# Attention on one core: pooled and local scores in turn on PE, even keys ahead of the normalising on GpSimd, tails in fours

## The chip, the cores and the metric

The kernel runs on one core of a Trainium2 chip. The metric is the device time of one execution in microseconds (us); lower is better.

## What is computed

Attention over 4 x 8 heads of 576 positions and 64 channels, then two dense layers over the 2304 tokens, all in float32. This change is in the attention.

```python
q_d = q.reshape(B, H, Sd, factor, D).mean(axis=3)      # factor = 4, Sd = 144; k_d, v_d too
out_d = sm_attn(q_d, k_d, v_d)                         # pooled: softmax over all 144 keys
out_up = np.repeat(out_d, factor, axis=2)
mask = np.abs(pos[:, None] - pos[None, :]) < factor    # local: keys at most 3 away
scores = np.where(mask, scale * np.matmul(q, k.transpose(0, 1, 3, 2)), -1000000000.0)
...
return (out_up + out_local).astype(np.float32)
```

The first layer is `(h * tanh(softplus(h))) @ w_out` with `h = x @ w_in` (512 to 2048 and back), the second a softmax-gated unit with layer norm (512 to 1024 and back).

## The kernel before, in words

Each engine has its program written out by hand, in the order in which it runs; semaphores tie them together. The attention works on 16 units, each a pair of heads of one batch: head 0 lies in partitions 0 to 63, head 1 in 64 to 127. All engines loop over u = 0 to 15 (PE and ACT two more), and the attention ends where PE takes up `hidden(0, ...)`, the first layer (L919).

- **SP** starts all loads, in one queue. In step s it sends for v of unit s - 2 (the values, 512 first positions, `v4`), in even s also the tails of two units (the last 64 positions, 16 partitions, `vt4`), then queries and keys of unit s (`qkT`, three buffers), then the windows of unit s - 3 (`vw`, the values of the local part). Each load first waits until its buffer is free: v until the values of two units earlier are pooled (`pool_v`), the tails until the pair before is (`pool_vt`).
- **POOL** (GpSimd) does in iteration u: `normalise_local(u - 1)` (L683, waits for `rden_ok`), queries of unit u + 1 and, if that is even, its keys (`pool_queries_keys`, L656 and L658: add pairs into `half_qk`, then add the halves), the values of unit u (`pool_values`, L666 and L668) and in even u the tails of u and u + 1 (`pool_two_tails`, L674 and L676). Steps of one pooling are chained by `own`, which waits for the engine's own last operation.
- **PE** in iteration u: `turn_local(u - 2)` (L851, needs that unit normalised), `turn_pooled(u - 2)` (L861, L866), `score_pooled(u)` (L819, six products of 64x144, one for each of three query blocks and two heads), `score_local(u)` (L832 masks, L838 twenty products of 64x64), then `value_pooled(u - 2)` (L878 with vd, L883 with the tails vdt) and `value_local(u - 2)` (L899). In units 0 and 1 the local scores come first. The local blocks are in two groups, jp = 0 and jp = 1 (the first and the second blocks); `half_rows(h, jp)` puts head h of the first blocks in the output rows of h, of the second blocks in those of the other head. The pooled scores go to the output rows of h.
- **DVE** in iteration u: pooled maxima (L1494, waits for `p_scored`), local maxima and subtraction (L1503, L1510, waits for `l_scored`), in even u the keys of the odd unit u + 1 (L1468), in odd u the eviction of a local output (L1532), sums (L1517) and the reciprocals `rden` (L1526). In iterations 3, 7 and 11 it also adds the pooled output (L1548), in 4, 8 and 12 it splits off a low part (L1554).
- **ACT**: copies of the turned parts (L1161, L1166), `normalise_pooled` (L1150), `exp_pooled` (L1141), `exp_local` (L1171), evictions.

After attention the layers run on PE without a gap; they are not touched.

## Time and profile before

| | us |
|---|---|
| median of 3 runs | 689.97 |
| lowest, highest | 688.26, 690.58 |
| the profiled execution | 683.98 |
| its span | 682.2 |
| PE busy in the span | 664.3 (97%) |
| DVE, ACT, POOL busy | 422.3, 325.7, 282.2 |

The profile is of one execution, whose own time is 683.98 us; busy time is per engine, and in 97% of the span PE works. The clock granted to PE was full (1.00) throughout. Start times below are counted from the start of the span.

### The profile page before, as it was taken

What the parts mean: (1) busy time and instruction counts of PE and PEld (TensorE: products, weight loads), DVE (VectorE), ACT (ScalarE), POOL (GpSimd) and SP (SyncE); (2) the same over time, 40 slices, a digit from 0 to 9 for tenths busy, and PEclk for the clock granted to TensorE, in tenths of its full rate; (3) what the DMA queues carried; (4) which work ended last, traced back from release to release, by engine and by line L of the source; (5) the groups of instructions that cost most, each with busy time, mean ns of one, the idle gap of its engine ahead of it and who ended that gap; (6) DMA issues with size and microseconds to landing.
All of it is one profiled execution on the core that took longest, in us unless ns stands there. A gap on an engine that the chain in (4) does not pass through costs nothing.

```text
span 682.2 us, 13003 instructions
## 1 busy us (share of the span) xinstructions
PE 664.3 (97%) x5002; PEld 570.3 (84%) x5002; DVE 422.3 (62%) x763; ACT 325.7 (48%) x687; POOL 282.2 (41%) x342
## 2 busy tenths in 40 slices
PE   5999999999999999999999999999999999999998
PEld 4777778888998989999899988888778888888886
DVE  7999859545765566555544322455787556855671
ACT  5999962343454366443442211137365454445432
POOL 6999803020795437554000000586355333542100
PEclk9999999999999999999999999999999999999999
DMA  8989791000000000000200001012100000000001
GB/s 263 255 269 271 184 369 38 0 1 1 1 0 1 1 1 1 1 1 1 62 2 1 1 0 61 1 32 63 31 16 16 31 32 31 1 32 31 32 17 47
DMA packets 26115, 37.54 MB, mean 55 GB/s; under 512 B 2512, under 2 KB 12742, under 8 KB 26054
## 3 DMA queue, kind: packets, MB, share of 16 engines
q1 hardware_dynamic: 26054, 36.71, 17.3%
q8 instruction: 40, 0.66, 0.4%
q14 instruction: 21, 0.17, 0.1%
HBM read 31.98 MB, written 4.72 MB: 54 GB/s over the span
## 4 chain that ended last, share of the span: by engine, by line
PE 91%; DVE 2%; ACT 2%; issue 2%; POOL 2%; DMA 0%; SPq 0%; ACTq 0%; POOLq 0%; DVEq 0%
PE psum L967 29%; PE psum L919 16%; PE psum L1080 14%; PE psum L1057 12%; PE psum L953 12%; PE psum L1066 2%; PE psum L819 1%; PE psum L851 1%; POOL prob L683 1%; PE psum L899 1%; PE psum L838 1%; PE psum L861 1%; PE psum L866 0%; ACT pprob L1141 0%; PE psum L878 0%
## 5 line engine op out<-in xcount | busy, mean ns | idle before, releaser
L967 PE MATMUL psum<-ghi,whi 128*128 128x512 f32 (+1 forms) x320 | 118.2, 370 | 0.0
L967 PE MATMUL psum<-glo,whi 128*128 128x512 f32 (+1 forms) x320 | 118.1, 369 | 0.0
L967 PE MATMUL psum<-ghi,wlo 128*128 128x512 f32 (+1 forms) x320 | 117.7, 368 | 0.0
L1216 ACT ACTIVATE g_sb<-psum 128x512 f32<-128x512 f32 (+1 forms) x48 | 25.3, 527 | 135.5 <-PE psum L919 134.7
L1598 DVE CAST ghi<-g_sb 128x512 fp32r<-128x512 f32 (+1 forms) x48 | 23.5, 490 | 102.2 <-PE psum L967 87.2
L919 PE MATMUL psum<-xhi,whi 128*128 128x512 f32 (+1 forms) x256 | 85.6, 365 | 0.5 <-ACT g_sb L1216 0.3
L1603 DVE TENSOR_TENSOR glo<-g_sb,ghi 128x512 fp32r<-128x512 f32 (+1 forms) x80 | 66.2, 828 | 19.6 <-ACT ghi L1242 18.0
L967 PEld LDWEIGHTS psum<-ghi,wlo 128*128 128x128 f32 x320 | 60.3, 189 | 10.3
L967 PEld LDWEIGHTS psum<-ghi,whi 128*128 128x128 f32 x320 | 60.5, 189 | 9.7 <-issue 0.4
L919 PE MATMUL psum<-xlo,whi 128*128 128x512 f32 (+1 forms) x192 | 68.0, 354 | 0.0
L967 PEld LDWEIGHTS psum<-glo,whi 128*128 128x128 f32 x320 | 60.5, 189 | 8.8
L953 PE MATMUL psum<-ahi,flo 128*128 128x256 f32 x224 | 63.4, 283 | 0.0
L953 PE MATMUL psum<-ahi,fhi 128*128 128x256 f32 x224 | 63.2, 282 | 0.0
L1080 PE MATMUL psum<-whi,lhi 128*128 128x512 f32 x144 | 56.4, 392 | 0.9 <-DVE llo L1757 0.9
L1080 PE MATMUL psum<-whi,llo 128*128 128x512 f32 x144 | 56.1, 389 | 0.0
L1080 PE MATMUL psum<-wlo,lhi 128*128 128x512 f32 x144 | 56.0, 389 | 0.0
L919 PEld LDWEIGHTS psum<-xhi,whi 128*128 128x128 f32 x256 | 48.3, 189 | 8.3 <-ACT g_sb L1216 0.4
L709 POOL TENSOR_TENSOR fsum<-wraw 128x256 f32<-128x256 f32 x16 | 12.3, 769 | 97.5 <-PE psum L953 35.9
L1057 PE MATMUL psum<-whi,yhi 128*128 128x512 f32 x126 | 50.8, 403 | 0.1
L1211 ACT ACTIVATE g_sb<-g_sb 128x512 f32<-128x512 f32 x32 | 20.2, 630 | 61.1 <-DVE g_sb L1654 61.1
L1057 PE MATMUL psum<-wlo,yhi 128*128 128x512 f32 x126 | 49.3, 391 | 0.0
L1057 PE MATMUL psum<-whi,ylo 128*128 128x512 f32 x126 | 49.1, 389 | 0.0
(175 smaller groups left out, 1607.2 us busy)
## 6 DMA issues: line engine op xcount, KB each, us to landing
wraw<-w_dram SPq DMA_DIRECT2D x12, 512.0 KB, 7.9
qkT<-qT_dram SPq DMA_DIRECT2D x16, 288.0 KB, 3.6
qkT<-kT_dram SPq DMA_DIRECT2D x16, 288.0 KB, 5.0
out_dram<-ob SPq DMA_DIRECT2D x18, 256.0 KB, 2.0
vw<-v_dram SPq DMA_DIRECT2D x15, 280.0 KB
v<-v_dram SPq DMA_DIRECT2D x16, 256.0 KB, 4.7
wraw<-w_dram SPq DMA_DIRECT2D x16, 256.0 KB, 7.1
b<-w_dram SPq DMA_DIRECT2D x4, 512.0 KB, 4.2
```

The lines of the kernel that those rows point to most:

```text
L683: nc.gpsimd.tensor_tensor(rows, rows, rden[:, par, 0:NB].unsqueeze(2).broadcast_to([P, NB, KW]), ALU.mult).then_inc(l_norm, 1)
L709: nc.gpsimd.tensor_tensor(to[:, 0], raw_block(j, 0, 1), raw_block(j, 0, 0), ALU.subtract).then_inc(ft_ok, 1)
L919: ins = nc.tensor.matmul(bank, a[:, kdx, :], b[:, kdx, 0:size], start=(kdx == 0 and n == 0), stop=(kdx == KD - 1 and n == 2))
L953: ins = nc.tensor.matmul(bank, a, b, start=(k == 0 and m == 0), stop=(k == KH - 1 and m == 2))
L967: ins = nc.tensor.matmul(psum[:, YB + m, 0:size], a[:, w], b[:, (t * F1 + f) % GR, 0:size], start=(f == 0 and n == 0), stop=(f == F1 - 1 a ...
L1057: ins = nc.tensor.matmul(bank, a[p % 2][:, n, k, :], b, start=(k == 0 and m == 0), stop=(k == KH - 1 and m == 2))
L1066: ins = nc.tensor.transpose(psum[:, T2B + c // 4, (c % 4) * P:(c % 4 + 1) * P], so[:, par, c * P:(c + 1) * P], ident[:])
L1080: ins = nc.tensor.matmul(bank, a[:, par, c, :], b[:, w], start=(c == 0 and n == 0), stop=(c == F2 - 1 and n == 2))
L1211: nc.scalar.activation(g_sb[:, f % HR, :], g_sb[:, f % HR, :], ACT.Mish).then_inc(g_ok, 1)
L1216: nc.scalar.activation(g_sb[:, f % HR, 0:size], psum[:, HB1 + f % HB, 0:size], ACT.Mish).then_inc(g_ok, 1)
L1598: nc.vector.tensor_copy(ghi[:, (t * F1 + f) % GR, 0:size], g_sb[:, f % HR, 0:size]).then_inc(ghi_ok, 1)
L1603: nc.vector.tensor_tensor(glo[:, (t * F1 + f) % GR, 0:size], g_sb[:, f % HR, 0:size], ghi[:, (t * F1 + f) % GR, 0:size].bitcast(F32), ALU. ...
```

## The change

On PE, units 2 to 15 get their scores from one function, `score_both`: masks of the second blocks, then pooled and local products of the second blocks in turn, then masks and products of the first blocks. It waits for all its inputs at its start. On GpSimd, keys are pooled apart from queries, and in odd iterations ahead of the normalising (in iteration 1 behind it); tails are pooled for four units at once (32 partitions each, 16 of them filled), so their products on PE use 32 rows instead of 64. The values of unit 1 are pooled in iteration 2, the first tails in iteration 1. SP sends for queries and keys ahead of the values; four tails are sent for at the start, and later two of them in each of the steps 3, 4, 7, 8, 11 and 12, the first two behind a wait for the tails before.

The diff. In `score_both` the inner functions `masked(jp)`, `local(i, jp, h)` and `pooled(b, h)` are left out; each issues the same product, with the same operands, as its line in `score_local` or `score_pooled`.

```diff
--- before.py
+++ after.py
@@ -42,6 +42,8 @@
 PR = HD + PB
 PS = 2 * HD
 PT = POOLED - P
+FOUR = 4
+QP = P // FOUR
 QPAD = (NPB - 1) * PB + HD
 
 SEQP = SEQ + 12
@@ -559,26 +561,33 @@
 
 
 
+            def load_tails(u, n):
+                for i in range(u, u + n):
+                    at = i % FOUR * QP
+                    tail = v_d[i][POOLF * P:SEQ].rearrange("(p t) c -> p (t c)", t=POOLF)
+                    sp.dma_start(vt4[at:at + PT, :], tail).then_inc(ld_vt4, 16)
+
             for s in range(UNITS + 3):
+                if s < UNITS:
+                    wait(sp, l_scored, s + 1 - RQ)
+                    wait(sp, p_scored, s + 1 - RQ)
+                    sp.dma_start(qkT[:, s % RQ, 0, 0:SEQ], qT_d[s]).then_inc(ld_qk[s % RQ], 16)
+                    sp.dma_start(qkT[:, s % RQ, 1, 0:SEQ], kT_d[s]).then_inc(ld_qk[s % RQ], 16)
                 if 1 < s < UNITS + 2:
                     u = s - 2
                     wait(sp, pool_v, u - 1)
                     sp.dma_start(v4[:, u % 2, :], v_d[u][0:POOLF * P].rearrange("(p t) c -> p (t c)", t=POOLF))\
                       .then_inc(ld_v4[u % 2], 16)
-                    if u == 0:
-                        sp.wait_ge(rest_ok, 2)
-                    if u % 2 == 0:
-                        wait(sp, pool_vt, u // 2)
-                        for h in range(2):
-                            tail = v_d[u + h][POOLF * P:SEQ].rearrange("(p t) c -> p (t c)", t=POOLF)
-                            sp.dma_start(vt4[h * HD:h * HD + PT, :], tail).then_inc(ld_vt4, 16)
-                if s < UNITS:
-                    wait(sp, l_scored, s + 1 - RQ)
-                    wait(sp, p_scored, s + 1 - RQ)
-                    sp.dma_start(qkT[:, s % RQ, 0, 0:SEQ], qT_d[s]).then_inc(ld_qk[s % RQ], 16)
-                    sp.dma_start(qkT[:, s % RQ, 1, 0:SEQ], kT_d[s]).then_inc(ld_qk[s % RQ], 16)
+                if s == 2:
+                    sp.wait_ge(rest_ok, 2)
+                    load_tails(0, FOUR)
                 if s > 2:
                     load_windows(s - 3)
+                if s > 2 and s % FOUR == FOUR - 1 and s + 1 < UNITS:
+                    sp.wait_ge(pool_vt, (s + 1) // FOUR)
+                    load_tails(s + 1, 2)
+                if s > 2 and s % FOUR == 0 and s < UNITS:
+                    load_tails(s + 2, 2)
                 if s in W_IN:
                     load_w_in(0, W_IN.index(s))
             for kdx in range(KD):
@@ -644,19 +653,24 @@
                                     base=0, pattern=[[KW, 2], [1, KW]], channel_multiplier=-1).then_inc(band_ok, 1)
             own(nc.gpsimd.memset(mhalf[:], -0.5))
 
-            def pool_queries_keys(u):
-                par = u % 2
+            def pool_two_adds(u, a, dst, ok):
+                halves = half_qk[:, a].rearrange("p (i r) -> p i r", r=2)
+                four = qkT[:, u % RQ, a, 0:SEQ].rearrange("p (i r) -> p i r", r=4)
+                own(nc.gpsimd.tensor_tensor(halves, four[:, :, 0:2], four[:, :, 2:4], ALU.add))
+                nc.gpsimd.tensor_tensor(dst[:, u % 2, 0:POOLED], halves[:, :, 0], halves[:, :, 1], ALU.add)\
+                  .then_inc(ok, 1)
+
+            def pool_queries(u):
                 pool.wait_ge(ld_qk[u % RQ], 32 * (u // RQ + 1))
                 wait(pool, p_scored, u - 1)
                 wait(pool, pool_q, u)
-                wait(pool, pool_k[0], (u + 1) // 2)
-                n = 1 if u % 2 else 2
-                halves = half_qk[:].rearrange("p a (i r) -> p a i r", r=2)
-                four = qkT[:, u % RQ, :, 0:SEQ].rearrange("p a (i r) -> p a i r", r=4)
-                own(nc.gpsimd.tensor_tensor(halves[:, 0:n], four[:, 0:n, :, 0:2], four[:, 0:n, :, 2:4], ALU.add))
-                for a, dst in enumerate((qd, kd)[:n]):
-                    nc.gpsimd.tensor_tensor(dst[:, par, 0:POOLED], halves[:, a, :, 0], halves[:, a, :, 1],
-                                            ALU.add).then_inc((pool_q, pool_k[0])[a], 1)
+                pool_two_adds(u, 0, qd, pool_q)
+
+            def pool_even_keys(u):
+                pool.wait_ge(ld_qk[u % RQ], 32 * (u // RQ + 1))
+                wait(pool, p_scored, u - 1)
+                pool.wait_ge(pool_k[0], u // 2)
+                pool_two_adds(u, 1, kd, pool_k[0])
 
             def pool_values(u):
                 par = u % 2
@@ -667,13 +681,13 @@
                 wait(pool, p_valued, u - 1)
                 nc.gpsimd.tensor_tensor(vd[:, par, :], half_v[:, 0:P], half_v[:, P:2 * P], ALU.add).then_inc(pool_v, 1)
 
-            def pool_two_tails(u):
-                two = u // 2
-                pool.wait_ge(ld_vt4, 32 * (two + 1))
-                wait(pool, pool_vt, two)
+            def pool_four_tails(u):
+                four = u // FOUR
+                pool.wait_ge(ld_vt4, 16 * FOUR * (four + 1))
+                wait(pool, pool_vt, four)
                 own(nc.gpsimd.tensor_tensor(half_vt[:], vt4[:, 0:2 * P], vt4[:, 2 * P:4 * P], ALU.add))
-                wait(pool, p_valued, u - 2)
-                nc.gpsimd.tensor_tensor(vdt[:, two % 2, :], half_vt[:, 0:P], half_vt[:, P:2 * P], ALU.add)\
+                wait(pool, p_valued, u - FOUR)
+                nc.gpsimd.tensor_tensor(vdt[:, four % 2, :], half_vt[:, 0:P], half_vt[:, P:2 * P], ALU.add)\
                   .then_inc(pool_vt, 1)
 
             def normalise_local(u):
@@ -684,14 +698,22 @@
                                         ALU.mult).then_inc(l_norm, 1)
 
             for u in range(UNITS + 1):
+                if u % 2 == 1 and 2 < u + 1 < UNITS:
+                    pool_even_keys(u + 1)
                 if u > 0:
                     normalise_local(u - 1)
-                if 0 < u + 1 < UNITS:
-                    pool_queries_keys(u + 1)
-                if u < UNITS:
+                if u == 1:
+                    pool_even_keys(2)
+                if u + 1 < UNITS:
+                    pool_queries(u + 1)
+                if u == 1:
+                    pool_four_tails(0)
+                elif u < UNITS:
+                    if u == 2:
+                        pool_values(1)
                     pool_values(u)
-                    if u % 2 == 0:
-                        pool_two_tails(u)
+                    if u > 0 and u % FOUR == 0:
+                        pool_four_tails(u)
                 if u == UNITS - 1:
                     pool.wait_ge(wi_hi, 2)
                     nc.gpsimd.tensor_tensor(first_low(1), in_piece(wraw, 1), first_high(1).bitcast(F32),
@@ -840,6 +862,49 @@
                                                    start=False, stop=(i == NP - 1))
                 ins.then_inc(l_scored, 1)
 
+            def score_both(u):
+
+                par = u % 2
+                qk = qkT[:, u % RQ].rearrange("p a s -> p (a s)")
+                pe.wait_ge(ld_qk[u % RQ], 32 * (u // RQ + 1))
+                pe.wait_ge(l_sub, u)
+                pe.wait_ge(pool_q, u + 1)
+                pe.wait_ge(pool_k[par], u // 2 + 1)
+                pe.wait_ge(p_exp, u)
+
...
+                masked(1)
+                for i in range(NP):
+                    for h in range(2):
+                        if i < NPB:
+                            ins = pooled(i, h)
+                            if (i, h) == (NPB - 1, 1):
+                                ins.then_inc(p_scored, 1)
+                        local(i, 1, h)
+                masked(0)
+                for i in range(NP):
+                    for h in range(2):
+                        ins = local(i, 0, h)
+                ins.then_inc(l_scored, 1)
+
@@ -860,7 +925,7 @@
                     at = b * PS
                     nc.tensor.transpose(turned[:, at:at + PR], pprob[0:PR, par, b, 0:P], ident[0:PR, 0:PR])
 
-                k0 = P - par * HD
+                k0 = P - u % FOUR * QP
                 for b in range(NPB):
                     at = TP1 + b * PS
                     ins = nc.tensor.transpose(turned[0:POOLED - k0, at:at + PR], pprob[0:PR, par, b, k0:POOLED],
@@ -871,8 +936,8 @@
                 par = u % 2
                 pe.wait_ge(p_copied, u + 1)
                 pe.wait_ge(pool_v, u + 1)
-                pe.wait_ge(pool_vt, u // 2 + 1)
-                half = slice(par * HD, (par + 1) * HD)
+                pe.wait_ge(pool_vt, u // FOUR + 1)
+                part = slice(u % FOUR * QP, (u % FOUR + 1) * QP)
                 for h in range(2):
                     rows = slice(h * HD, (h + 1) * HD)
                     nc.tensor.matmul(turned[rows, OD0:OD0 + POOLED], vd[:, par, rows], pprobT[:, 0, :, h, :],
@@ -880,8 +945,8 @@
 
                 for h in range(2):
                     rows = slice(h * HD, (h + 1) * HD)
-                    ins = nc.tensor.matmul(turned[rows, OD0:OD0 + POOLED], vdt[half, u // 2 % 2, rows],
-                                           pprobT[half, 1, :, h, :], start=False, stop=True)
+                    ins = nc.tensor.matmul(turned[rows, OD0:OD0 + POOLED], vdt[part, u // FOUR % 2, rows],
+                                           pprobT[part, 1, :, h, :], start=False, stop=True)
                 ins.then_inc(p_valued, 1)
 
             def value_local(u):
@@ -978,12 +1043,11 @@
                 if u >= LATE:
                     turn_local(u - LATE)
                     turn_pooled(u - LATE)
-                if u < UNITS:
-                    if u >= FIRST:
-                        score_pooled(u)
+                if u < FIRST:
                     score_local(u)
-                    if u < FIRST:
-                        score_pooled(u)
+                    score_pooled(u)
+                elif u < UNITS:
+                    score_both(u)
 
                 if u == UNITS:
                     pe.wait_ge(l_sub, UNITS)
```

The order of instructions. First POOL, from the values of unit 1 (before) and the tails of units 0 to 3 (now) to the normalising of unit 2. In the names half_v and vd are values, half_vt and vdt tails, qd and kd pooled queries and keys, `prob<-prob,rden` is a normalising. Before:

```order
L666 TENSOR_TENSOR half_v<-v_58 128x256 [waits pool_v,ld_v4_1]
L668 TENSOR_TENSOR vd<-half_v 128x128 [waits pool_own]
L683 TENSOR_TENSOR prob<-prob,rden 128x640 [waits rden_ok]
L656 TENSOR_TENSOR half_qk<-qkT 128x288 [waits pool_q,pool_k0,p_scored,ld_qk0]
L658 TENSOR_TENSOR qd<-half_qk 128x144 [waits pool_own]
L666 TENSOR_TENSOR half_v<-v_58 128x256 [waits pool_v,ld_v4_0]
L668 TENSOR_TENSOR vd<-half_v 128x128 [waits p_valued,pool_own]
L674 TENSOR_TENSOR half_vt<-vt_59 128x256 [waits pool_vt,ld_vt4]
L676 TENSOR_TENSOR vdt<-half_vt 128x128 [waits pool_own]
L683 TENSOR_TENSOR prob<-prob,rden 128x640 [waits rden_ok]
```

and now:

```order
L688 TENSOR_TENSOR half_vt<-vt_59 128x256 [waits ld_vt4]
L690 TENSOR_TENSOR vdt<-half_vt 128x128 [waits pool_own]
L697 TENSOR_TENSOR prob<-prob,rden 128x640 [waits rden_ok]
L659 TENSOR_TENSOR half_qk<-qkT 128x288 [waits pool_q,p_scored,ld_qk0]
L660 TENSOR_TENSOR qd<-half_qk 128x144 [waits pool_own]
L680 TENSOR_TENSOR half_v<-v_58 128x256 [waits pool_v,ld_v4_1]
L682 TENSOR_TENSOR vd<-half_v 128x128 [waits pool_own]
L680 TENSOR_TENSOR half_v<-v_58 128x256 [waits pool_v,ld_v4_0]
L682 TENSOR_TENSOR vd<-half_v 128x128 [waits p_valued,pool_own]
L659 TENSOR_TENSOR half_qk<-qkT 128x288 [waits pool_k0,p_scored,ld_qk1]
L660 TENSOR_TENSOR kd<-half_qk 128x144 [waits pool_own]
L697 TENSOR_TENSOR prob<-prob,rden 128x640 [waits rden_ok]
```

The values of unit 1 come behind the first normalising of these (unit 1) and directly ahead of those of unit 2; there are no tails between; and the keys of unit 4 stand ahead of the normalising of unit 2 instead of behind it.

Second, SP's queue from the last window load of unit 0 on (v_58 values, vt_59 tails). Before:

```order
L537 DMA vw<-v_dram 6x5x128
L566 DMA v_58<-v_dram 128x512 [waits pool_v]
L574 DMA vt_59<-v_dram 16x512 [waits pool_vt]
L574 DMA vt_59<-v_dram 16x512
L578 DMA qkT<-qT_dram 128x576 [waits p_scored,l_scored]
L579 DMA qkT<-kT_dram 128x576
L537 DMA vw<-v_dram 112x5x128
```

and now:

```order
L539 DMA vw<-v_dram 6x5x128
L568 DMA vt_59<-v_dram 16x512 [waits pool_vt]
L568 DMA vt_59<-v_dram 16x512
L574 DMA qkT<-qT_dram 128x576 [waits p_scored,l_scored]
L575 DMA qkT<-kT_dram 128x576
L579 DMA v_58<-v_dram 128x512 [waits pool_v]
L539 DMA vw<-v_dram 112x5x128
```

The values of unit 2 were next behind the windows; now they are behind two tails, which wait for `pool_vt`, and behind queries and keys of unit 4.

## Rows read from the trace of the kernel before

**Rows 1.** Windows, 20 us of attention and 20 us of the first layer.

```profile
core 0: us, PE busy (x) PEld busy (x) DVE busy (x) ACT busy (x) POOL busy (x), PEclk, DMA share, GB/s
40.00:60.00 20.00, 18.45 (x504) 15.57 (x495) 18.78 (x40) 18.80 (x60) 19.21 (x28) 1.00 0.87 249
120.00:140.00 20.00, 20.00 (x90) 16.57 (x89) 9.40 (x18) 6.36 (x12) 0.00 (x0) 1.00 0.01 1
```

**Rows 2.** Timeline of POOL: start us, us, engine, line, operation, out<-in, count.

```profile
47.40 0.82 POOL L668 TENSOR_TENSOR vd<-half_v 128x128 f32<-128x128 f32 x1
48.19 0.73 POOL L674 TENSOR_TENSOR half_vt<-vt 128x256 f32<-128x256 f32 x1
...
49.41 1.26 POOL L683 TENSOR_TENSOR prob<-prob,rden 128x640 f32<-128x640 f32 x1
50.62 1.15 POOL L656 TENSOR_TENSOR half_qk<-qkT 128x576 f32<-128x576 f32 x1
...
52.23 0.42 POOL L658 TENSOR_TENSOR kd<-half_qk 128x144 f32<-128x144 f32 x1
...
53.83 1.26 POOL L683 TENSOR_TENSOR prob<-prob,rden 128x640 f32<-128x640 f32 x1
55.05 0.67 POOL L656 TENSOR_TENSOR half_qk<-qkT 128x288 f32<-128x288 f32 x1
...
56.17 0.73 POOL L666 TENSOR_TENSOR half_v<-v 128x256 f32<-128x256 f32 x1
```

**Rows 3.** Timeline of DVE over units 9 to 11.

```profile
53.31 0.24 DVE L1526 RECIPROCAL rden<-dsum 128x13 f32<-128x13 f32 x1
53.75 0.61 DVE L1494 TENSOR_REDUCE psum<-psum 128x3 f32<-128x432 f32 x1 [0.19 <-PE psum L819]
...
58.12 0.24 DVE L1526 RECIPROCAL rden<-dsum 128x13 f32<-128x13 f32 x1
58.28 0.55 DVE L1494 TENSOR_REDUCE psum<-psum 128x3 f32<-128x432 f32 x1
...
63.02 0.24 DVE L1526 RECIPROCAL rden<-dsum 128x13 f32<-128x13 f32 x1
```

**Rows 4.** Timeline of PE, its iteration 11.

```profile
55.72 0.77 PE L851 MATMUL psum<-ident,prob 128*128 128x128 f32 x5
...
57.00 0.71 PE L819 MATMUL psum<-kd,qd 64*64 64x144 f32 x8
...
57.53 0.42 PE L819 MATMUL psum<-kd,qd 64*64 64x144 f32 x4
...
58.60 0.47 PE L878 MATMUL psum<-pprobT,vd 128*64 128x144 f32 x4
59.00 0.34 PE L883 MATMUL psum<-pprobT,vdt 64*64 64x144 f32 x2
59.01 0.38 PE L899 MATMUL psum<-probT,vw 64*64 64x58 f32 x5
...
59.96 0.77 PE L851 MATMUL psum<-ident,prob 128*128 128x128 f32 x5
```

**Rows 5.** Timeline of SP's queue, the load of unit 2's values.

```profile
10.69 0.36 SPq L566 DMA_DIRECT2D v<-v_dram  x1
```

**Rows 6.** Timeline of POOL, first and third normalising.

```profile
10.87 1.26 POOL L683 TENSOR_TENSOR prob<-prob,rden 128x640 f32<-128x640 f32 x1
...
20.09 1.26 POOL L683 TENSOR_TENSOR prob<-prob,rden 128x640 f32<-128x640 f32 x1
```

**Rows 7.** Timeline of DVE, pooled maxima of unit 4.

```profile
24.88 0.62 DVE L1494 TENSOR_REDUCE psum<-psum 128x3 f32<-128x432 f32 x1 [0.16 <-PE psum L819]
```

**Rows 8.** The loads of tile v, from issue to landing.

```profile
DMA to landing us min/median/max: 3.4/4.7/7.3
```

**Rows 9.** Timeline of POOL, normalising of unit 12.

```profile
68.66 1.26 POOL L683 TENSOR_TENSOR prob<-prob,rden 128x640 f32<-128x640 f32 x1
```

**Rows 10.** Timeline of PE, end of attention, where unit 14 is turned.

```profile
80.52 0.33 PE L899 MATMUL psum<-probT,vw 64*64 64x58 f32 x7 [1.00 <-issue]
80.78 0.77 PE L851 MATMUL psum<-ident,prob 128*128 128x128 f32 x5
```

16 lines of the change are left out of this document (added).

## The prediction

> **What bounds the kernel now.** I read the windows first, then the timelines of GpSimd (POOL), VectorE (DVE) and PE through a few units, then the start and the end of attention. The windows say where a change of attention can count: in the first layer PE is busy 20.00 of 20 us, in attention no engine is, but POOL has 19.21, ACT 18.80, DVE 18.78 and PE 18.45 [rows 1]. After attention PE never waits for long, so the program ends earlier or later by the amount by which PE gets earlier or later to the turning of unit 14, at 80.78 us [rows 10].
>
> Inside attention POOL is the pace-maker. Its operations follow one another with no idle time; normalising starts at 49.41 for unit 8 and 68.66 for unit 12, so four units take 19.25 us [rows 2, 9]. DVE is close behind: the reciprocals of unit 10 end at 58.12 + 0.24 = 58.36, 4.61 after that unit's pooled maxima started (53.75), those of unit 11 at 63.26, 4.90 later, and each time POOL comes for them within 0.3 us [rows 3]. Now the maxima of an even unit wait for PE, and PE for POOL: the even keys are ready 3.24 us after normalising began (49.41 to 52.65), and the maxima start 4.34 after it [rows 2, 3].
>
> **GpSimd's work.** From start to start: normalising N 1.22 (53.83 to 55.05); halving and pooling one of queries or keys 1.12 (55.05 to 56.17); tails T 1.22 (48.19 to 49.41), and values V the same, as the shapes are [rows 2]. Before, the even unit's half over both took 1.15 and its two second steps 0.4 each, 2.03 together (50.62 to 52.65); apart they are 2 x 1.12 = 2.24, so the split costs 0.2 per even unit. Tails by fours save 1.22 per four units. Per four units that is 0.4 more and 1.2 less: POOL needs 0.8 less, 18.4. DVE can't follow so far: 18.78 of 20 busy is 18.1 of 19.25, and its two short waits for ACT's exponentials stay, so 18.1 to 18.7 is its floor (estimate). Were work alone the limit, 0.5 to 1.1 per four units would be won.
>
> **The new loop.** The even keys now stand ahead of the normalising, and PE turns a unit (which needs it normalised) ahead of the next scores. So the order adds 1.12 to the wait of the turning. From a normalising's start to the maxima two units on: 1.26, 0.05 to PE, 1.28 turning (55.72 to 57.00), 0.95 pooled scores (57.00 to 57.95), 0.04 = 3.58 [rows 2, 4]. Every fourth unit has the tails just ahead of the even keys. From the reciprocal before them: 0.07, N + query + V + T 4.78, a block of 0.37 (vd at 47.40 took 0.82 where a slightly wider kd took 0.42 [rows 2]; this recurs in such a unit, with DVE's work beside it), even keys 1.12, 3.58 to the maxima, 4.61 and 4.90 to the two next reciprocals: 19.43. That is 0.18 more than the 19.25 of now. So I expect the saved work to become a wait of POOL for reciprocals ahead of the tails, with a late normalising behind them: little won or lost in the steady part, +0.4 over the two such loops from unit 4 to 12.
>
> **The start.** SP is one queue. In its step 3 it now waits for the first tails to be pooled, before unit 4's queries and keys and unit 2's values are sent for. The first normalising is at 10.87 [rows 6]; behind it stand even keys, queries and tails, 1.22 + 1.12 + 1.12 + 1.22, so the wait ends at 15.55. Then come two tails and two other loads, 0.36 [rows 5] to 0.5 us each, and unit 2's values go out at about 17.25 (10.69 before [rows 5]). Values land 3.4 to 4.7 after issue, 7.3 at worst [rows 8]: at 20.7 to 22.0, I take 21.3 because the queue has run empty. POOL wants them at 15.55 + N + query + V = 19.1, and unit 4's keys and the normalising of unit 2 stand behind them: it starts at 21.3 + 1.22 + 1.12 = 23.65 instead of 20.09 [rows 6]. Unit 4's maxima follow at +3.58 = 27.2 instead of 24.88 [rows 7]: 2.3 late. Windows for unit 1 are sent for later too, and come at about the same time as this, so they hide. POOL then reaches unit 4's normalising at 23.65 + 3.56 + 0.4 (a block) + 4.78 + 0.37 + 1.12 = 33.9, and two loops bring unit 12's to 72.8, 4.1 after the 68.66 of now [rows 9].
>
> **PE.** The pooled scores use the diagonal pairs of row and column halves, and of the local ones the second blocks use the other two. Both groups already overlap, and the diagonal ones carry pooled, mask and first blocks whatever the order: 57.00 to 58.60, 1.60 [rows 4]. In turn they may shorten this by up to 0.15, or delay the last pooled product by up to 0.2, if the loads between them cost time; I take nothing for both. The new waits ahead of the pooled scores (scores subtracted, local queries and keys) are fulfilled before PE comes to them in either order.
>
> The tail product is the other edit on PE. Its tile goes from 64 rows to 32. Now the switch from vd (128 rows) to vdt (64) takes 58.60 to 59.00, 0.40, and then the local values start beside vdt at 59.01, in the same 64 x 64 shape [rows 4]. With 32 rows both sides of vdt differ, so I charge a second 0.35 per unit (bounds 0, and the 0.40 of the row). The Trainium skill (TensorEngine Tiling (Array Packing), Key Properties) says that changing the tiling mode, not just the tile, drains TensorE; the trace agrees, with the 0.40 between 58.60 and 59.00 and none before 59.01. Inside the loop PE has that to spare: two units take 9.2 of 9.6. At the end it has not.
>
> **The end.** There are no tails at unit 14 any more, and POOL is no longer last. PE is: 1.31 after unit 12's normalising starts it turns unit 12, and two iterations of 4.24 (55.72 to 59.96 [rows 4]) + 0.35 later it turns unit 14, at 72.8 + 10.5 = 83.3. Now it is 80.78, and that holds a pause of 1.00 inside the local values which no semaphore explains [rows 10]. +2.5 if it doesn't recur, +3.5 if it does. I take +2.9.
>
> **The sum.** Start +2.3 at unit 4's maxima; +1.4 more by unit 12's normalising, which is the late place behind the tails, and +0.4 of the loops; end -1.2 with what PE adds: +2.9. The profiled execution is 683.98 us for a span of 682.2, and becomes 686.9; the median of the runs shown, 689.97, lies 6.0 above it, and becomes 692.9.
>
> **Rivals.** (1) *The start stays late and the steady part runs at DVE's pace.* If normalising never gets late behind the tails (shorter turning, POOL blocked less) a loop is 18.7, two win 1.1, and the missing tails of unit 14 another 1.0: +2.3 - 2.1 = +0.2, 690.2. For it: POOL's work is 18.4. Against: the sum of 19.43 has only measured terms. Chance 0.30. (2) *Faster.* The mechanism is the same relief of POOL, without the late values. It decides at POOL's second values in its iteration 2: if unit 2's values are there by 19.1, nothing is lost, and -2.1 to -2.4 remains, 687.7. Against it: issue at 17.25 would need a landing in 1.9 us, and the quickest was 3.4 [rows 8]; only an earlier end of the first tails would do. Chance 0.12. (3) *Starved loads.* In steps 7 and 11 SP again waits for the tails, and the values of units 6, 10 and 14 are sent behind that wait, about 3 us later than now, with some 5 us left against landings of 4.7 and up to 7.3 [rows 8]. One more microsecond each: +3 on the forecast, 695.9. Chance 0.13. The forecast has 0.45. That the interleaving does nothing for the time is part of all four.
>
> **How the numbers follow.** About 0.3%, 2.07 us, is what can be told from no change: below 687.9 faster, above 692.0 slower. The forecast's own range is 691.3 to 694.5 (values landing at 3.4 or 4.7, pause or none, second switch 0 or 0.40), some four fifths of it above 692.0. With rival 3, that gives slower 0.52; faster 0.12; the rest, rival 1 and the lower part of the forecast, 0.36. The range of 8 in 10 leaves out rival 2 and the far part of rival 3: 688.2 to 695.6.
>
> **What would show it.** Right: POOL idle before unit 2's values by some 2 us, released by a load; normalising of unit 2 near 23.6, of unit 12 near 72.8; short idles of POOL on reciprocals before the iterations with tails; maxima of even units 3.6 after normalising instead of 4.3; vdt and the local values no longer starting together; pooled scores ended 0.95 after their start. Wrong: no load in POOL's idle time at the start, four units in 18.7, or unit 14 turned by 81.

## The result and the profile after

| | before | after |
|---|---|---|
| median, runs on the same chip | 687.1 (9 runs) | 692.98 (9 runs) |
| lowest, highest | 684.39, 690.58 | 690.16, 695.74 |
| the profiled execution | 683.98 | 690.16 |
| its span | 682.2 | 688.3 |
| pooled maxima of unit 4 | 24.88 | 28.64 |
| normalising of units 4, 8, 12 | 30.13, 49.41, 68.66 | 35.21, 54.89, 75.17 |
| turning of unit 14 | 80.78 | 86.54 |

Ratio 1.0101, 95% interval 1.0078 to 1.0123: slower by 6.9 us (5.4 to 8.5). The two medians of the table are only 5.9 apart. Three of the nine runs of before are those shown ahead of the prediction (689.97, 688.26, 690.58), among the slowest; the other six have a median of 686.2, and from there it is 6.8.

The forecast's sign and its 692.9 us came true, but the second only by chance. It was +2.9 on the profiled execution, where +6.2 was measured; and before itself, in this comparison, has a median of 687.1 and not the 689.97 from which the forecast started. A loss of 0.4% was foreseen, and 1.0% came.

The windows of the changed kernel first, with the columns of [rows 1].

```profile
core 0: us, PE busy (x) PEld busy (x) DVE busy (x) ACT busy (x) POOL busy (x), PEclk, DMA share, GB/s
40.00:60.00 20.00, 18.65 (x468) 14.92 (x466) 18.32 (x39) 18.23 (x58) 17.74 (x27) 1.00 0.92 248
120.00:140.00 20.00, 20.00 (x90) 16.57 (x89) 11.79 (x22) 6.50 (x12) 0.00 (x0) 1.00 0.00 0
```

POOL has become lighter, 17.74 of 20 us instead of 19.21, and nothing was won by it. The first layer is as full as it was, so the difference again stands in the turning of unit 14, +5.76 of the +6.1 in the span. Here is the end of attention on PE (timeline, as in [rows 10]), with three more places where PE stopped or was stopped. The last number in brackets is the idle time before a row, and behind the arrow stands what ended it; "issue" means that the profile shows nothing that ended it.

```profile
12.58 0.77 PE L916 MATMUL psum<-ident,prob 128*128 128x128 f32 x5 [1.61 <-POOL prob L697]
...
14.99 0.47 PE L879 MATMUL psum<-maskb,identb 64*64 64x320 bf16 x2 [1.07 <-POOL qd L660]
...
17.97 0.45 PE L943 MATMUL psum<-pprobT,vd 128*64 128x144 f32 x2
...
54.11 0.68 PE L884 MATMUL psum<-qkT 64*64 64x64 f32 x17 [1.06 <-issue]
...
81.74 0.46 PE L964 MATMUL psum<-probT,vw 64*64 64x58 f32 x17 [1.01 <-issue]
...
86.54 0.66 PE L916 MATMUL psum<-ident,prob 128*128 128x128 f32 x4
```

Next come three views of the start: SP's queue from step 3 on (compare [rows 5], where unit 2's values go out at 10.69), POOL's timeline ([rows 6, 9]), and the maxima of unit 4 on DVE ([rows 7]).

```profile
16.02 0.79 SPq L568 DMA_DIRECT2D vt<-v_dram  x2
16.91 0.37 SPq L574 DMA_DIRECT2D qkT<-qT_dram  x1
17.32 0.43 SPq L575 DMA_DIRECT2D qkT<-kT_dram  x1
17.80 0.43 SPq L579 DMA_DIRECT2D v<-v_dram  x1
```

```profile
10.05 0.72 POOL L680 TENSOR_TENSOR half_v<-v 128x256 f32<-128x256 f32 x1 [1.56 <-DMA v<-v_dram]
...
15.54 0.46 POOL L690 TENSOR_TENSOR vdt<-half_vt 128x128 f32<-128x128 f32 x1
...
22.23 0.73 POOL L680 TENSOR_TENSOR half_v<-v 128x256 f32<-128x256 f32 x1 [2.67 <-DMA v<-v_dram]
...
24.57 1.26 POOL L697 TENSOR_TENSOR prob<-prob,rden 128x640 f32<-128x640 f32 x1
25.79 1.11 POOL L659 TENSOR_TENSOR half_qk<-qkT 128x288 f32<-128x288 f32 x1
...
68.56 1.26 POOL L697 TENSOR_TENSOR prob<-prob,rden 128x640 f32<-128x640 f32 x1 [0.98 <-DVE rden L1590]
...
71.28 0.73 POOL L680 TENSOR_TENSOR half_v<-v 128x256 f32<-128x256 f32 x1 [0.33 <-DMA v<-v_dram]
...
75.17 1.26 POOL L697 TENSOR_TENSOR prob<-prob,rden 128x640 f32<-128x640 f32 x1
```

```profile
28.64 0.62 DVE L1558 TENSOR_REDUCE psum<-psum 128x3 f32<-128x432 f32 x1 [1.04 <-PE psum L890]
```

What to see: the first tails are pooled at 15.54 + 0.46 = 16.00, SP takes up its queue at 16.02, and unit 2's values leave at 17.80. POOL then stands for 2.67 until they are there. Later waits for values are small: four after 23 us, of 0.23 to 0.56 (0.33 at 71.28 is one).

The same stretch in windows, changed kernel, then the kernel before, shows a thing that the forecast hadn't in it.

```profile
14.00:16.00 2.00, 1.01 (x25) 1.04 (x29) 0.42 (x2) 2.00 (x6) 1.84 (x5) 0.71 0.02 6
16.00:18.00 2.00, 2.00 (x40) 1.81 (x34) 0.78 (x2) 0.50 (x4) 1.92 (x3) 0.50 0.17 42
18.00:20.00 2.00, 2.00 (x54) 1.53 (x53) 1.88 (x4) 1.23 (x7) 1.48 (x3) 0.94 0.94 288
```

```profile
14.00:16.00 2.00, 1.77 (x59) 1.74 (x60) 1.17 (x5) 1.98 (x5) 1.92 (x4) 1.00 0.93 297
16.00:18.00 2.00, 2.00 (x56) 1.74 (x55) 1.97 (x5) 1.63 (x8) 1.92 (x4) 1.00 1.10 277
```

While SP waits the DMA engines are empty (0.02 instead of 0.93). In the same stretch the clock granted to PE falls to 0.50, which is 1.2 GHz, after PE had waited 1.61 for the first normalising and 1.07 for unit 2's queries. Unit 2's scores take 14.99 to 17.97, 2.98 us, instead of 1.60 [rows 4].

What brings the clock down there isn't shown, and it isn't SP's wait alone. Between 12 and 18 us seven of the fourteen traces of this document have a window of 2 us at 0.50 to 0.56: the changed kernel, e2, e3, e4, e7, e9 and e11. Three of them, e2, e7 and e9, have no wait of SP in step 3, and e9 is the kernel before with nothing but the scores in turn. PE's two waits don't decide it either: they are 0.94 and 1.07 both in e3, where the clock fell to 0.53, and in e5, where it stayed at 1.00; in the kernel before they are 1.34 and 0.70, at 1.00.

### The profile page after: what moved, and what is told of

It reads as the page before. It is cut to its first block, busy times and chain, and to the rows that moved or that the text cites. A ratio compares the mean times of both kernels' runs of the same rounds, so it can differ in the third digit from the quotient of the medians.

```text
span 688.3 us, 12986 instructions
## 1 busy us (share of the span) xinstructions
PE 667.7 (97%) x5002; PEld 571.2 (83%) x5002; DVE 424.4 (62%) x763; ACT 326.1 (47%) x687; POOL 278.3 (40%) x341
## 4 chain that ended last, share of the span: by engine, by line
PE 86%; POOL 8%; DVE 2%; issue 2%; DMA 1%; ACT 1%; SPq 0%; POOLq 0%; ACTq 0%; DVEq 0%
PE psum L1032 29%; PE psum L984 16%; PE psum L1144 13%; PE psum L1121 12%; PE psum L1018 12%; POOL prob L697 2%; PE psum L1130 2%; POOL half_qk L659 2%; POOL half_v L680 1%; DMA v<-v_dram 1%; POOL vd L682 1%; POOL qd L660 1%; PE psum L916 1%; PE psum L964 0%; POOL half_vt L688 0%
```

## The experiments

All ratios are to the kernel before, run beside them.

| run | what it is | ratio | 95% interval |
|---|---|---|---|
| after | the changed kernel | 1.0101 | 1.0078 to 1.0123 |
| e1_late_tails | without SP's wait ahead of the values | 1.0038 | 1.0020 to 1.0057 |
| e2_two_tails | tails by twos | 1.0043 | 1.0025 to 1.0061 |
| e3_keys_behind | even keys behind the normalising | 1.0076 | 1.0053 to 1.0098 |
| e4_scores_apart | scores not in turn | 1.0104 | 1.0076 to 1.0133 |
| e5_start_mended | e1, and values ahead of queries on SP | 1.0029 | 1.0007 to 1.0052 |
| e6_mended_filler | e5, and filler products on PE | 1.0013 | 0.9997 to 1.0030 |
| e7_combined | e5, and even keys behind the normalising | 1.0031 | 1.0012 to 1.0050 |
| e8_only_keys | before, with keys split and even keys ahead | 1.0015 | 0.9994 to 1.0036 |
| e9_only_scores | before, with scores in turn | 1.0004 | 0.9984 to 1.0025 |
| e10_only_fours | before, with tails by fours and keys split | 1.0025 | 1.0005 to 1.0045 |
| e11_changed_filler | the changed kernel, with filler products | 1.0078 | 1.0055 to 1.0101 |
| e12_before_filler | before, with filler products | 0.9997 | 0.9973 to 1.0020 |

### SP's wait (e1)

```diff
-                if s > 2 and s % FOUR == FOUR - 1 and s + 1 < UNITS:
-                    sp.wait_ge(pool_vt, (s + 1) // FOUR)
-                    load_tails(s + 1, 2)
                 if s > 2 and s % FOUR == 0 and s < UNITS:
-                    load_tails(s + 2, 2)
+                    sp.wait_ge(pool_vt, s // FOUR)
+                    load_tails(s, FOUR)
```

> The changed kernel, but SP sends for the next four tails in one piece at the end of steps 4, 8 and 12, behind the values and windows of that step, instead of two of them behind a wait at the end of steps 3, 7 and 11. Theory A (the wait in SP's step 3 makes unit 2's values late, and the delay lasts): GpSimd no longer idles 2.7 us for them, the pooled maxima of unit 4 start near 25.1 instead of 28.6 us, and 3 to 3.5 us of the 6 to 7 are given back: ratio to before 1.003 to 1.006. Theory B (the start is made up anyway; the loss is in the loops and in PE's pauses): the start moves, the end does not, ratio 1.008 or more.

Measured: 688.79 against 685.97, ratio 1.0038. SP's queue, and POOL's timeline, of this kernel:

```profile
13.04 0.43 SPq L579 DMA_DIRECT2D v<-v_dram  x1
...
15.75 1.72 SPq L568 DMA_DIRECT2D vt<-v_dram  x4
```

```profile
19.45 0.73 POOL L678 TENSOR_TENSOR half_v<-v 128x256 f32<-128x256 f32 x1
...
21.80 1.26 POOL L695 TENSOR_TENSOR prob<-prob,rden 128x640 f32<-128x640 f32 x1
```

Unit 2's values go out at 13.04 instead of 17.80, POOL pools them at 19.45 without a wait for a load, and unit 2 is normalised at 21.80 instead of 24.57. Between the two ratios lie 0.63%, 4.3 us: the wait of SP for the tails is the larger part of the loss. The mean granted clock of the runs, too, is nearer to that of before (0.9973; before 0.9982, changed kernel 0.9942). The two kernels were not run in the same comparison, so the 4.3 us have the width of both intervals, some 2 us on either side.

The profiled execution shows less of it. Unit 4's maxima are at 25.95 (near 25.1 was expected, 28.64 in the changed kernel), but unit 14 is turned at 84.55 instead of 86.54, 2.0 earlier. It holds a wait of 1.07 for values at 69.25, and the clock granted from 76 to 78 us was 0.50.

### Tails by twos (e2)

In the changed kernel the loads, the pooling and the products of the tails are those of before; SP's new order of queries and values, the early keys and the scores in turn stay.

Of its edit, the part in POOL's loop:

```diff
-                if u == 1:
-                    pool_four_tails(0)
-                elif u < UNITS:
-                    if u == 2:
-                        pool_values(1)
+                if u < UNITS:
                     pool_values(u)
-                    if u > 0 and u % FOUR == 0:
-                        pool_four_tails(u)
+                    if u % 2 == 0:
+                        pool_two_tails(u)
```

> The changed kernel with tails by twos again (loads, pooling, 64-row products), everything else as changed. GpSimd then has 18.9 us of own work per four units and 0.8 of blocks, 19.7, more than the 19.25 of before. Theory A: the start is as before (maxima of unit 4 at 25 to 25.5), the loops are 19.7, ratio 1.002 to 1.004. Theory B (keys ahead of the normalising, scores in turn or pauses cost the most): ratio 1.007 or more.

Measured: ratio 1.0043. This also takes away SP's wait, and by the ratio it gives back as much as e1 does. Its loops of four units take 19.8 us each, as foreseen (normalising at 34.83, 54.62 and 74.41). Its trace does not show the start that was expected: unit 4's maxima are at 28.41, not at 25 to 25.5. In this execution the granted clock was 0.64, 0.50, 0.50 and 0.65 in the windows from 14 to 22 us, and POOL waited 1.87 for the reciprocals of unit 3, until 28.57. How the start ran in its other executions isn't known. Once SP's wait is away, fours and twos can't be told apart (1.0038 against 1.0043): the pooling of tails saved on POOL bought nothing that can be measured.

### Even keys behind the normalising (e3)

```diff
-                if u % 2 == 1 and 2 < u + 1 < UNITS:
-                    pool_even_keys(u + 1)
                 if u > 0:
                     normalise_local(u - 1)
-                if u == 1:
-                    pool_even_keys(2)
+                if u % 2 == 1 and u + 1 < UNITS:
+                    pool_even_keys(u + 1)
```

> The changed kernel with the even keys behind the normalising again (still apart from the queries). Theory A: the start stays late by 3.5 us or more, and a loop gets 0.2 shorter (maxima 4.5 after normalising against 1.12 + 3.58): ratio 1.008 to 1.010. Theory B (the late normalising behind the tails is most of the loss): ratio 1.006 or less.

Measured: ratio 1.0076, 1.7 us less than the changed kernel, though the intervals overlap. In the trace unit 2 is normalised at 23.30 instead of 24.57, since the keys of unit 4 (1.12) no longer stand between the late values and it. That piece is a cost of the order only where POOL has been held up; e7 below puts the same edit on the mended start. The ratio fell between the two theories (1.008 to 1.010, and 1.006 or less). The start did stay late (maxima of unit 4 at 28.38), but the trace does not show loops shorter by 0.2: the two take 20.67 and 19.71, together 40.4, against 40.0 in the changed kernel.

### Scores apart (e4)

```diff
-                if u < FIRST:
-                    score_local(u)
-                    score_pooled(u)
-                elif u < UNITS:
-                    score_both(u)
+                if u < UNITS:
+                    if u >= FIRST:
+                        score_pooled(u)
+                    score_local(u)
+                    if u < FIRST:
+                        score_pooled(u)
```

> The changed kernel with pooled scores ahead of all local scores again. My theory: no difference in time, since scoring takes 1.60 to 1.62 us in both orders: ratio 1.009 to 1.011 as for the changed kernel. Rival: taking turns brings PE's pauses of 1.0 us (four or more of them against one before) or the low clock at unit 2; then they go, and the ratio is 1.007 or less.

Measured: ratio 1.0104, against 1.0101 with the scores in turn. No difference can be told. Its profiled execution was an unlucky one (granted clock 0.989 on average, a pause of 1.50 us on PE ending at 24.80), and its start times are therefore not compared. The low clock at unit 2 (0.50 from 16 to 18 us) came without the turns as well, and the ratio did not fall, so the rival falls.

### Start mended altogether (e5), filler products (e6), keys behind (e7)

e5 is e1 with SP's loads of queries and keys behind that of the values again:

```diff
-                if s < UNITS:
-                    ...
-                    sp.dma_start(qkT[:, s % RQ, 1, 0:SEQ], kT_d[s]).then_inc(ld_qk[s % RQ], 16)
                 if 1 < s < UNITS + 2:
                     ...
+                if s < UNITS:
+                    ...
+                    sp.dma_start(qkT[:, s % RQ, 1, 0:SEQ], kT_d[s]).then_inc(ld_qk[s % RQ], 16)
```

> The kernel of e1 (tails of four sent for behind windows), and SP sends for values ahead of queries and keys again, as before the change. What e1 left of the start is GpSimd's 1.6 us wait for unit 0's values and 0.5 to 1.1 us waits for later ones. Theory A: those waits go, and another 1 us is given back: ratio 1.002 to 1.003. Rival (the rest is the loops' order and the low clock): 1.0035 to 1.0045.

e6 adds four products that nobody reads, ahead of unit 2's scores:

```diff
                 elif u < UNITS:
+                    if u in (2,):
+                        for i in range(4):
+                            nc.tensor.matmul(psum[:, OB, 320:448], ident[:], ident[:], start=True, stop=True)
                     score_both(u)
```

> The kernel of e5 with four products of the identity with itself (0.2 us each at full clock) on PE, written to unused columns, ahead of unit 2's scores, so that PE works where it waits for unit 2's queries. Clock theory: the clock, which fell to its low level at about 15 us in four of five profiles of changed kernels and in none of before, stays at 1.00, unit 2's scores take 1.6 us instead of 3, and the time falls by 1 to 1.7 us against e5. Rival: the clock falls as often, or later, and the time is that of e5 within 0.5 us.

e7 is e5 with the edit of e3.

> The kernel of e5 with the even keys behind the normalising, as in e3. The start is as before, and GpSimd's work is 18.5 us per four units, with a loop of 19.1 behind the tails by my sum, no tails at unit 14. Theory A (the loop of late normalising is real, 0.3 us and more per four units): faster than e5 by 1 to 2 us, ratio 1.000 or below. Rival (position of the keys hardly matters; the shorter work of GpSimd does not reach the end): ratio that of e5.

Measured: 688.29, 687.03 and 688.86 against 686.26; ratios 1.0029, 1.0013 and 1.0031. In e5 the maxima of unit 4 are at 25.28, 0.4 behind those of before, and the first normalising at 10.54: the 1.56 us for which POOL stood ahead of unit 0's values are gone. Yet some 2 us stay. The keys ahead of the normalising or behind it make no difference now (1.0029, 1.0031). e6 had a granted clock of 1.00 in 7 of its 12 runs, e5 in 2 of 12; its ratio is lower by 1.1 us, which the intervals allow but don't prove. Nor do the traces: unit 2's scores had the full clock in both, in e5 without filler, so there was nothing there for the filler to mend.

### One edit at a time on the kernel before (e8, e9, e10)

e8 splits queries and keys and puts the even keys ahead of the normalising, in the kernel before (the two functions are those of the changed kernel):

```diff
+                if u % 2 == 1 and 2 < u + 1 < UNITS:
+                    pool_even_keys(u + 1)
                 if u > 0:
                     normalise_local(u - 1)
-                if 0 < u + 1 < UNITS:
-                    pool_queries_keys(u + 1)
+                if u == 1:
+                    pool_even_keys(2)
+                if u + 1 < UNITS:
+                    pool_queries(u + 1)
```

> The kernel before with one part of the change alone: keys apart from queries, and ahead of the normalising (tails by twos, scores and loads as before). GpSimd's work grows by 0.4 per four units, blocks stay. If GpSimd is the limit: loops of 19.7 and the end 1.3 to 2 us later, ratio 1.002 to 1.003. If the late turning costs more than the work: 1.004 or more. If PE waiting less for queries and keys helps: below 1.001.

e9 puts `score_both` there for units 2 to 15 and nothing else (the diff of e4, turned round).

> The kernel before with the changed kernel's scoring on PE from unit 2 on, nothing else. Theory: the order of pooled and local products costs and brings nothing by itself; scores apart in the changed kernel (ratio 1.0104) stood where the changed kernel did (1.0101). Ratio 0.999 to 1.0015; pooled maxima 0.97 after the scoring's start, as in the changed kernel, against 0.95. Rival: in turn, the last pooled product comes later where the local loads are slow, and each iteration of DVE grows by 0.02 to 0.1: +0.3 to +1.4 us in 14 units, ratio 1.0005 to 1.002. If it is above 1.0025, the interleaving is a cost that the pair of runs before hid.

e10 has tails by fours, loaded as in e1, with keys split but behind the normalising. Against the kernel before, on SP and on POOL:

```diff
+                if s > 2 and s % FOUR == 0 and s < UNITS:
+                    sp.wait_ge(pool_vt, s // FOUR)
+                    load_tails(s, FOUR)
...
-                    if u % 2 == 0:
-                        pool_two_tails(u)
+                    if u > 0 and u % FOUR == 0:
+                        pool_four_tails(u)
```

> The kernel before with tails by fours only (products of 32 rows, the loads of four tails sent in one piece behind the windows in steps 4, 8 and 12, values of unit 1 pooled in iteration 2), and the keys apart from the queries but behind the normalising. Scores and SP's order of values, queries and keys as before. The combined kernel (e7) is this with the scores in turn, and was at 1.0031 (1.0012 to 1.0050). Theory A: scores in turn are worth nothing, so 1.002 to 1.004 again (+1.5 to +2.5 us), and what tails by fours cost lies in the longer blocks of four units. Theory B: most of e7's time came from scores in turn on top of fours: below 1.001. Normalising of unit 12 near 72.5 under A, near 70.5 under B.

Measured: 1.0015, 1.0004 and 1.0025. Only the last is told from 1, and barely. In the trace of e8 the four units take 19.63 and 19.62 (19.7 was foreseen), and unit 14 is turned at 82.22, 1.4 behind the kernel before: the split keys ahead of the normalising cost what POOL's work grew by, where the ratio can't tell it. The scores in turn are worth nothing that can be measured (0.3 us, -1.1 to +1.7). For e10 its theory A holds by the ratio. Its normalising of unit 12, at 70.48, is what theory B foresaw (70.5) and not A (72.5), but its profiled execution took 686.26, 1.4 less than its median, so between the two it stays open. Even so it turns unit 14 at 82.61, 1.8 behind the kernel before. All of the pieces taken singly come to 0.44%, and all together without the wait (e5) to 0.29%; both fit in the intervals.

### Filler in the changed kernel and in the one before (e11, e12)

The same four products, by the diff of e6, ahead of unit 2's scores in each: in the changed kernel (e11) and in the kernel before (e12).

> The changed kernel with four products of 128 x 128 on PE (ident by ident, into a part of PSUM nobody reads) ahead of unit 2's scores, and nothing else. Theory: part of the changed kernel's time is the lower clock in unit 2's scores (14.99 to 17.97, 3.0 us instead of 1.6, granted 0.50 to 0.71), worth 1.3 us there; the filler keeps the clock up, mean granted clock of the fast runs rises from 0.994 to 0.996 or more, and the ratio falls from 1.0101 to 1.007 to 1.0085. Rival: unit 2's normalising waits for its values (landing near 24) whatever PE does, so the clock there costs nothing and the ratio stays at 1.0095 to 1.0105, with the norm of unit 2 at 24.5 again.

> The kernel before with the same four products ahead of unit 2's scores. The kernel before has two levels of time: 684.7 to 685.4 where its mean granted clock is 1.0, 686.6 to 686.8 where it is 0.998, in 18 of some 56 runs 1.0. Theory: a low stretch early in attention makes most of the second kind, and the filler removes some: ratio 0.998 to 0.9995, a mean clock of 1.0 in over half of the runs. Rival: the low stretches come elsewhere (a pause of PE in a unit, the end of attention), and the four products add nothing but 0.2 us: 0.9995 to 1.0005, with the clock's levels as often as before.

Measured: e11 691.49 against 686.31, ratio 1.0078; e12 686.04, ratio 0.9997. The timeline of PE in e11, filler first:

```profile
14.46 1.86 PE L1052 MATMUL psum<-ident 128*128 128x128 f32 x8
16.24 0.32 PE L879 MATMUL psum<-maskb,identb 64*64 64x320 bf16 x2
...
17.86 0.34 PE L943 MATMUL psum<-pprobT,vd 128*64 128x144 f32 x2
```

The ratio of e11 fell as the clock theory said, but the trace doesn't bear out the way. Here the clock was down before the filler ran (0.67 in the window from 12 to 14, 0.50 from 14 to 16), the filler took 1.86 us at the low level (1.07 in e6 and e12 at the full one), and the scores, now 1.62, ended at 17.86: 0.11 earlier than without it. Unit 2 was normalised at 24.22, again behind its values. The mean clock rose only from 0.9942 to 0.9953, and the intervals of the two ratios overlap. So what the low clock at unit 2 costs the changed kernel isn't settled; the rival, that late values hide it, is what this one trace shows.

Where no late values hide it, it does cost. In e9, the kernel before with the scores in turn, the clock granted was 0.50 from 14 to 16, and POOL waits for unit 2's reciprocals (normalising of unit 2, 20.09 in the kernel before):

```profile
21.02 1.26 POOL L683 TENSOR_TENSOR prob<-prob,rden 128x640 f32<-128x640 f32 x1 [0.80 <-DVE rden L1568]
```

On the kernel before the filler does nothing (4 of its 12 runs had a mean clock of 1.00, and the theory wanted over half). None of the kernels tried is quicker than the kernel before.

### What PE's pauses are

No run was made for this; the twelve traces and the two of the kernels answer it together. The forecast had to leave open a pause of PE that no semaphore explains [rows 10]. Three such stand in the changed kernel (1.06 and 1.01 above, and 0.95 ending at 32.94), and e9 and e12 had the longest. Their timelines of PE, e9 first:

```profile
73.86 0.71 PE L942 MATMUL psum<-probT,vw 64*64 64x58 f32 x27 [2.81 <-issue]
```

```profile
79.03 0.57 PE L899 MATMUL psum<-probT,vw 64*64 64x58 f32 x25 [3.39 <-issue]
```

Below is the view of the DMA queues in quarters of a microsecond: e9 from 71.00 to 71.25, then e12 from 76.25 to 76.50, then the changed kernel from 51.25 to 51.50 (queue, kind: packets, MB, share of the 16 engines).

```profile
q1 hardware_dynamic: 74, 0.04, 106.8%
q8 instruction: 1, 0.02, 30.6%
```

```profile
q1 hardware_dynamic: 45, 0.06, 109.5%
q8 instruction: 1, 0.02, 30.6%
```

```profile
q1 hardware_dynamic: 36, 0.07, 93.5%
q8 instruction: 1, 0.02, 31.4%
```

Queue q8 brings packets of instructions of 16,384 bytes each, 40 of them in a run. It is PE's queue: from one packet to the next PE starts 266 instructions on average in attention, where the packets come 5.5 us apart, and 248 behind it, where they come 22 us apart (kernel before). DVE's numbers, for one, don't keep so even: 14 and 29.

In the fourteen traces PE has 17 pauses of 0.85 us or more in attention without a releaser. If all of PE's records in the trace are counted from the start (products, weight loads and those of its sequencer), 15 of the 17 stand exactly behind record 961, 1217, 1473, 1729, 1985, 3009, 3265 or 3521. All of these lie a multiple of 256 instructions apart, so they are the seams of a program that comes in pieces of 256 instructions; at one piece a packet that is 64 bytes an instruction. Each of the 15 ends 2.3 to 3.2 us after the start of the last packet before it (the three views above show that packet for e9, e12 and the pause ending at 54.11). The rest of the crossings say the same: from record 705 to record 3521 there are 12 seams, so 168 crossings in the fourteen traces. The second packet belongs to the first of these seams, the third to the next and so on, and PE never passed a seam sooner than 2.3 us after the start of its packet. So at these places PE runs out of program and goes on when the next piece has come, through DMA engines that carry other packets at the same time (q1 above, 93.5 to 109.5%). In e9 and e12 the packet itself started late: PE stood at the seam already.

The other two of the 17, 1.50 ending at 24.80 in e4 and 1.03 ending at 24.14 in e11, lie at no seam. They stand ahead of unit 1's local values, and the windows of unit 1, for which PE waits there, were sent for only at 18.35 and 18.12, behind SP's wait. The profile has no landings of windows, so this reading is argued and not shown. Pauses shorter than 0.85 without a releaser are of more than one kind: 0.65 and 0.40 ahead of the pooled scores recur in every loop of the kernel before, and at no seam.

The Trainium skill (Runtime: NRT & Kernel Launch, Instruction fetch mechanics) says that the sequencer fetches its program in 16 KiB blocks and that crossing a block is mostly hidden. The trace agrees with the size, 16,384 bytes a packet, and with "mostly": 141 of the 168 crossings cost less than 0.25 us. It leaves out the 15 that cost 0.89 to 3.39. Why one packet starts late and another doesn't was not tried.

A pause can cost twice. In e9, after 2.81, the clock granted is 0.50 between 75 and 77; in e12, after 3.39, it is 0.60 from 79 to 82; in e5, after 1.28, it is 0.50 from 80 to 82. It need not: after 2.52 in e7 and 1.99 in e5, and after the three pauses of the changed kernel, it stayed at 1.00.

## Why the forecast was right in its mechanism and short in its size

**The start: right, and 1.3 us short.** POOL stood before unit 2's values, released by a load (2.67 where "some 2" was foreseen), and e1 shows that SP's wait is the cause. The issue came at 17.80 and not 17.25, because the tails' end was 16.00 and not 15.55 (unit 0's values had held POOL for 1.56: SP's new order, which the forecast had not priced; in e5 it is gone). The landing came 4.4 after issue, within 3.4 to 4.7, later than the 4.05 taken "because the queue has run empty". Normalising of unit 2 therefore stands at 24.57 against 23.65. Unit 4's maxima are 4.07 behind it, against 3.58, of which 0.44 is the halving of the queries at 25.79, 1.11 long instead of 0.67; a block of this kind was in the sum, but only further on. Normalising of unit 4: 35.21 against 33.9.

**The loops: the sum was right, the pauses were not in it.** The first two loops take 19.68 and 20.28, foreseen was 19.43 each. The second pays for the pause of 1.06 that ends at 54.11, in the scores of unit 10, after which DVE waits 0.73 for PE. The kernels with fours and without a pause in the loop come out close to the sum: 19.43 in e10, 19.45 in e5, 19.70 in e7 (normalising of unit 8 to unit 12). Their loops from unit 4 to 8 have a pause inside (0.91 in e10) or just before (1.99 in e5, 2.52 in e7), and take 20.63, 21.29 and 21.37. POOL's idle time is where it was foreseen, on reciprocals ahead of the iteration with tails (0.98 at 68.56). So the saved work did turn into a wait, and four units became 0.2 longer or more. Unit 12 is normalised at 75.17 against 72.8.

**PE: the second switch was mis-sized.** The changed kernel's iteration 11:

```profile
57.57 0.32 PE L879 MATMUL psum<-maskb,identb 64*64 64x320 bf16 x2
...
58.26 0.28 PE L890 MATMUL psum<-kd,qd 64*64 64x144 f32 x1
...
59.19 0.47 PE L943 MATMUL psum<-pprobT,vd 128*64 128x144 f32 x4
59.58 0.46 PE L948 MATMUL psum<-pprobT,vdt 32*64 32x144 f32 x4
59.97 0.80 PE L964 MATMUL psum<-probT,vw 64*64 64x58 f32 x40
60.71 0.55 PE L916 MATMUL psum<-ident,prob 128*128 128x128 f32 x3
```

The switch is there, 0.39 between L948 and L964, and the two no longer start together [rows 4]. But the local values behind it take 0.74 (59.97 to 60.71) instead of the 0.95 that they took beside vdt (59.01 to 59.96), so the iteration grew by 0.17 (4.41 against 4.24), not 0.35. The pooled scores end 0.97 after the start of the scoring (58.26 + 0.28 - 57.57), before 0.95: "nothing" for the interleaving was right, and e4 and e9 show it.

**The end.** From unit 12's normalising to the turning of unit 14 it took 11.37; 10.5 was foreseen without a pause, 11.5 with one of 1.00. One of 1.01 came.

**The sum.** The turning of unit 14 came at 86.54, foreseen 83.3: 3.2 late, of it 1.3 at the start, 1.1 in the loops and 0.9 at the end. About 1.9 of these are the two pauses; of the 1.3, 0.9 are the later issue and landing of unit 2's values, 0.4 the longer halving of queries. What the sum lacked is on PE: it charged stalls of loads and blocks of POOL, and for a pause of PE 0.4 at one place, where this execution had two that counted. Whether the change makes such pauses more frequent isn't shown; before has them too, at the same seams.

**The rivals.** (1) fell: no loop was 18.7. (2) fell: values landed at 22.2, not by 19.1. (3), starved loads at later units, is there but small: waits for values of 0.23 to 0.56, not one microsecond each (one of 1.07 in e1). What no rival had was a lower clock. Over its runs, the kernel before needs 684.5 to 685.1 where its mean granted clock is 1.000 and 687.9 to 688.3 where it is 0.995 (medians of such runs in three comparisons). The changed kernel's mean is 0.9942, before's is 0.9976 to 0.9982 in the three. At 2.9 to 3.7 us for 0.005, the difference would be 2 to 3 us of the 6.9. This is an estimate, and not the price of the clock alone: in e9 and e12 a long pause came first and the low clock followed, so runs with a low clock are also runs with such pauses. e1, which raised the clock to 0.9973, can't part the late start from the clock either.

## What to carry over

When a load is put behind a wait in a queue, price everything that the queue would have sent in that time: here SP waited for one small buffer and sent nothing from 11.3 to 16.0, and that made some 4 of the 6.9 us (4.3, uncertain by some 2). Without it the change was still 0.3 to 0.4% slower (e1, e5), and which of its parts costs that stays open. Work saved on the busiest engine counts only as far as the next one follows; DVE stood 2% behind POOL, so the most that could be won was small while each new wait was paid. And one trace is one execution: e2's and e10's traces disagree with their own medians on where the time went, so a place in a trace says how a time can arise, and only the runs say how much it is.

## What had not been expected of the hardware

- PE pauses of 0.9 to 3.4 us exactly at seams 256 instructions apart, ending 2.3 to 3.2 us after the start of a packet of the instruction queue, seen in 11 of 14 traces, also in the kernel before. They may make a part of the spread from run to run; that was not measured.
- The clock granted to PE fell to 0.50 after waits of 1.61 and 1.07 us close to each other (changed kernel, 12 to 18 us), and unit 2's scores took 2.98 us instead of 1.60. Like waits can go either way: those of 0.94 and 1.07 were followed by 0.53 in e3 and by 1.00 in e5. In attention's steady part the granted clock was 1.00 with PE busy 18.65 of 20 us.
- To switch to products on 32 rows and from them costs 0.39 each, as much as the switch to 64 rows before (0.40), but 40 local values that then have PE for themselves take 0.74 instead of 0.95 beside another product.
